# A Silu table load ahead of the output copies, and packed transposes one block later, in an attention and two-layer feed-forward kernel

## The chip, the core and the metric

The kernel runs on one core of one Trainium2 chip. The metric is the device time of one execution in microseconds (us). The core has TensorE (PE in the profile, the matrix engine), VectorE (DVE), ScalarE (ACT), GpSimd (POOL) and SyncE (SP, which here only issues DMAs). Each engine works through its own instructions in order, and waits on semaphores that other engines raise.

## What is computed

```python
def sm_attn(qq, kk, vv):
    s = scale * np.matmul(qq, kk.transpose(0, 1, 3, 2))
    s = s - np.max(s, axis=-1, keepdims=True)
    a = np.exp(s)
    a = a / (np.sum(a, axis=-1, keepdims=True) + 1e-09)
    return np.matmul(a, vv)
p_packed = sm_attn(p, k, v)             # 32 packed rows attend to 576 tokens
out = sm_attn(q, p_packed, p_packed)    # 576 tokens attend to the 32 packed rows
...
rms = np.sqrt(np.mean(x * x, axis=-1, keepdims=True) + 1e-06)
xn = x / rms * rms_g
g = xn @ w_gate
silu = g * (1.0 / (1.0 + np.exp(-g)))
val = xn @ w_val
x = silu * val @ w_out                  # first feed-forward layer, d_ff 1536
...
h = x @ w_in
g = np.maximum(h, 0.0) + alpha * np.minimum(h, 0.0)
return g @ w_out                        # second layer, d_ff 2048
```

There are 8 batches, 8 heads, 576 tokens of 64 dims a head, so 4608 tokens of model width 512. Everything is float32.

## The kernel before, in words

There are two stages. Stage one (about 50 to 810 us of the trace, after a prologue for batch 0) runs attention and the first feed-forward layer. Stage two runs the second layer, and the change does not touch it.

Stage one is a sequence of 16 token tiles, two halves (half 0 and half 1, 288 tokens each) for each of the 8 batches. A tile runs over 12 blocks f = 0 to 11 of 128 hidden units. Each wide product is made of three matmul passes (high and low parts, lines 476 to 478). For a block PE does

- the gate product: 6 matmuls, an_hi/an_lo against m_hi/m_lo, into one PSUM bank;
- the value product: 6 more into another bank;
- the down product of block f - 2: 12 matmuls, h_hi/h_lo against ow_hi/ow_lo, into four banks.

After the 12 blocks two more down products (of blocks 10 and 11) finish a tile. ACT makes Silu of the gate (line 851) once the gate product is done; DVE multiplies it with the value product (line 1050, called the multiply below); ACT rounds the result to h_hi (line 857); DVE makes the rest h_lo (line 1053). There is one gate bank and one value bank, so PE may start the gate product of block f only when Silu of f - 1 is done (`silu_done`), and the value product of f only when the multiply of f - 1 is done (`h32_done`). At the end of a tile DVE copies two output banks (line 1061) and ACT two (lines 865 and 867).

Beside tile (batch b, half) the attention of batch b + 1 is made in small pieces. The order is written out by hand in three tables, PE_PLACES, DVE_PLACES and ACT_PLACES. A key such as (0, "between", 4) means: in half 0, at block 4, at the hook "between". On PE "after" lies between the value product of a block and the down product, and "between" behind the down product. On DVE and ACT "within" lies ahead of the block's first instruction, "after" behind the multiply or Silu, and "between" behind h_lo or h_hi. The last batch has nothing beside it. The pieces that matter here:

- `exp0`, `exp1` on ACT: Exp over the packed scores, behind Silu of block 3 in half 0. `norm0`, `norm1` on DVE divide by the sums (line 932 last).
- `turn_a01` on PE: 8 transposes of those probabilities (line 510), which wait for `norm1` (`a_normed`). They fill banks 2 and 3. `turn_a0` on ACT (line 773) and `turn_a1` on DVE (line 938) copy them out. `turn_a2` on PE, behind the down product of block 5, is 2 more transposes into bank 2, and waits for the copy of `turn_a0` (`at_act`).
- `probs` on ACT in half 0 at block 11: Exp of the second attention. `sums0`, `probs0`, `turn_p0` on DVE at the start of half 1 finish it.
- `fold0` to `fold5` and `x0` to `x3` in half 1: PE products for the next batch's m and x. `x0` (line 575) waits for `m_lo_done`, which DVE raises at line 1010. ACT makes m_hi at line 818.
- `rsqrt0`, `rsqrt1` on ACT in half 1: Ln and Exp.

Exp and Ln use another ACT function table than Silu. A table is loaded by an ACT_TABLE_LOAD instruction; where the program has none, one is put in front of the first activation that needs the other table (the loads at lines 851, 764 and 783). At each of the first 14 tile ends Exp was the last function used, so a load for Silu stands in front of the next tile's first Silu.

Of the kernel before, what the change touches and what calls it, by code (L numbers as in the profile page):

```python
# [40 lines left out]
PE_PLACES = {  # L41
    (0, "ready", 1): ["scores0_ready"], (0, "after", 1): ["scores0"],
    (0, "ready", 2): ["scores1_ready"], (0, "after", 2): ["scores1"],
    (0, "between", 4): ["turn_a01"], (0, "between", 5): ["turn_a2"], (0, "between", 6): ["packed"],
    (0, "after", 7): ["turn_packed"],
# [8 lines left out]
}  # L54
DVE_PLACES = {
    (0, "between", 2): ["max0", "max1"], (0, "between", 3): ["norm0"],
    (0, "within", 4): ["norm1"], (0, "within", 5): ["turn_a1"], (0, "within", 7): ["packed"],
# [8 lines left out]
}  # L66
ACT_PLACES = {
    (0, "between", 1): ["scores0"], (0, "between", 2): ["scores1"], (0, "after", 3): ["exp0", "exp1"],
    (0, "after", 5): ["turn_a0"], (0, "within", 6): ["turn_a2"],
    (0, "within", 8): ["packed"], (0, "after", 11): ["probs"],  # L70
# [3 lines left out]
}  # L74
FILLERS = {"scores0": 3, "scores1": 1, "turn_a01": 2, "packed": 1, "turn_packed": 1, "tokens0": 1, "tile": 6}

# [1 line left out]
def build(nc, q_t, k_t, v_s, p_t, w1_gv, w1_o, w2, rms_g, alpha, out_t):  # L78
# [3 lines left out]
    with ExitStack() as ctx:  # L82
# [127 lines left out]
        def first(c):  # L210

            return isinstance(c, int) and c == 0
# [540 lines left out]
        def _(act):  # L753
            def scores_copy(c, h):

                act.wait_ge(scores_mm, 2 * c + h + 1)
                if h == 0:
                    reached(act, a2n_done, 2 * c)
                nc.scalar.copy(a_sb[:, :, h * HALF:(h + 1) * HALF], scores_ps).then_inc(scores_out, 1)

            def scores_exp(c, g):

                act.wait_ge(bias1_done, GROUPS * c + g + 1)
                nc.scalar.activation(a_sb[:, g, :], a_sb[:, g, :], ACT.Exp, bias=bias1[:, g:g + 1],
                                     scale=SCALE, accum_out=sum1[:, g:g + 1]).then_inc(exp1_done, 1)

            def turn_a(c, t):
                if t == 0:
                    reached(act, mean_mm, 2 * c)
                act.wait_ge(at_mm, 3 * c + t + 1)  # L770
                rows = slice(0, P) if t == 0 else slice(LAST, P)
                dst = a_t[rows, 2 * t:min(2 * t + 2, CHUNKS), :]
                nc.scalar.copy(dst.rearrange("p j n -> p (j n)"), at_ps[t][rows, :]).then_inc(at_act, 1)

            def packed(c):
                act.wait_ge(ppt_mm, c + 1)
                reached(act, s2_mm, 2 * c)
                reached(act, ppg_done, c)
                nc.scalar.copy(flat(pp_t[:]), ppt_ps).then_inc(ppt_copied, 1)

            def probs(c):
                act.wait_ge(sub2_done, 2 * c + 2)
                nc.scalar.activation(flat(e2[:].rearrange("p h g s -> p h (g s)")), flat(e2[:].rearrange("p h g s -> p h (g s)")),
                                     ACT.Exp, scale=SCALE).then_inc(exp2_done, 2)

            def probs_half(c, h):
                act.wait_ge(sub2_done, 2 * c + h + 1)
                nc.scalar.activation(e2[:, h], e2[:, h], ACT.Exp, scale=SCALE).then_inc(exp2_done, 1)

            def tokens_out(c, i):  # L790
                act.wait_ge(x_mm, 4 * c + i + 1)
                if i == 2:
                    act.wait_ge(mean_mm, 2 * c + 1)
                at = x_bank(c, i)
                nc.scalar.activation(sq[:, 2 * (i % 2):2 * (i % 2) + 2, :], psum[:, at:at + 2, 0:HALF],
                                     ACT.Square).then_inc(squared, 1)

            def rsqrt(c, h):

                nc.scalar.preload_act_table_set("natural_log_exp_and_others")  # L800
                act.wait_ge(mean_copied, 2 * c + h + 1)
                reached(act, a2n_done, 2 * c + h - 1)
                nc.scalar.activation(rinv[:, h, :], mean_sb[:, h, :], ACT.Ln).then_inc(log_done, 1)
                act.wait_ge(log_done, 2 * c + h + 1)
                nc.scalar.activation(rinv[:, h, :], rinv[:, h, :], ACT.Exp, scale=-0.5).then_inc(rsqrt_done, 1)

            def split(c, h):
                act.wait_ge(a2n_done, 2 * c + h + 1)
                if not first(c) and h == 0:
                    act.wait_ge(hidden_mm, NF1 * (2 * c - 1))  # L810
                nc.scalar.copy(an_hi[:, h], a2[:, h]).then_inc(an_hi_done, 1)

            def folded(c, j):
                act.wait_ge(m_mm, NF1 // 2 * c + j + 1)
                if not first(c):
                    act.wait_ge(hidden_mm, NF1 * (2 * c - 1) + 2 * j + 2)
                for e in range(2):
                    nc.scalar.copy(m_hi[:, 2 * j:2 * j + 2, e, :],
                                   psum[:, m_bank(c, j) + e, :].rearrange("p (f n) -> p f n", f=2)).then_inc(m_hi_done, 1)

            def beside(c, name):
                if name in ("scores0", "scores1"):
                    scores_copy(c, int(name[-1]))
                if name in ("exp0", "exp1"):
                    scores_exp(c, int(name[-1]))
                if name in ("turn_a0", "turn_a2"):
                    turn_a(c, int(name[-1]))
                if name == "packed":
                    packed(c)
                if name == "probs":  # L830
                    probs(c)
                if name in ("probs0", "probs1"):
                    probs_half(c, int(name[-1]))
                if name[0] == "x":
                    tokens_out(c, int(name[1:]))
                if name[:4] == "fold":
                    folded(c, int(name[4]))
                if name in ("rsqrt0", "rsqrt1"):
                    rsqrt(c, int(name[-1]))
                if name == "split0":  # L840
                    split(c, 0)

            def tile(b, half, at):
                n = 2 * b + half
                for f in range(NF1):
                    at("within", f)
                    act.wait_ge(gate_mm, NF1 * n + f + 1)
                    if f >= SLOTS:

                        act.wait_ge(h_lo_done, NF1 * n + f - 2)  # L850
                    nc.scalar.activation(act_sb[:, f % SLOTS, :], gate_ps, ACT.Silu).then_inc(silu_done, 1)  # L851
                    at("after", f)
                    act.wait_ge(h32_done, NF1 * n + f + 1)
                    if f >= SLOTS:

                        act.wait_ge(down_mm, NF1 * n + f - 2)
                    nc.scalar.copy(h_hi[:, f % SLOTS, :], act_sb[:, f % SLOTS, :]).then_inc(h_hi_done, 1)  # L857
                    at("between", f)
                    if half == 0 and f == 1:
                        split(b, 1)  # L860


                act.wait_ge(y_stored, 16 * n + 16)
                act.wait_ge(out_mm, (KC - 1) * n + 3)
                nc.scalar.copy(y_sb[:, 2, :], y_ps(2)).then_inc(y_act, 1)
                act.wait_ge(down_mm, NF1 * n + NF1)
                nc.scalar.copy(y_sb[:, 3, :], y_ps(3)).then_inc(y_act, 1)  # L867
                at("end", 0)

            nc.scalar.preload_act_table_set("natural_log_exp_and_others")  # L870
            for name in ("scores0", "scores1", "exp0", "exp1", "turn_a0", "turn_a2", "packed", "probs0", "fold0", "probs1",
                         "fold1", "fold2", "x0", "x1", "fold3", "rsqrt0", "x2", "x3", "split0", "fold4", "fold5", "rsqrt1"):
                beside(0, name)
            tiles_of_a(act, tile, beside)


# [247 lines left out]
```

## Time and profile before

| | |
|---|---|
| median of 3 runs | 1603.03 us (1602.67 to 1603.18) |
| profiled execution | 1600.78 us, of it the span of the trace 1599.0 us |
| PE busy | 1563.8 us, 98% of the span |
| DVE busy | 730.1 us, 46% |
| ACT busy | 489.3 us, 31% |
| POOL busy | 206.8 us, 13% |
| chain of work that ended last | PE 91%, DVE 4%, ACT 4%, issue 1% |
| PE clock granted | 0.995 on the mean; 8 tenths in the first of 40 slices, 9 or more after |

The engines are asynchronous, so a busy share says who works most, and not yet where time is lost. The lost time is in the idle stretches of PE, and the view that groups waits names who ended each. Start times are counted from the span's start. A matmul's listed length overlaps the next one's; in steady work one of 288 columns starts every 0.13 us.

### The profile page before, as it was taken

How to read it: one execution, taken by the hardware profiler on the slowest of the kernel's cores; microseconds unless marked ns; L12 is line 12 of the kernel's file. 1: busy time of each engine (PE TensorE's matmuls, PEld its weight loads, DVE VectorE, ACT ScalarE, POOL GpSimd, SP SyncE). 2: the span in 40 equal slices, each digit the busy share in tenths (PEclk: the TensorE clock that was granted, in tenths of full speed). 3: DMA queues.
4: the chain of work that ended last, by engine and by line, in shares of the span. 5: the costliest groups of instructions: out<-in, count | busy, mean ns of one | idle time of the engine just before them, and what ended most of it. 6: DMA issues, size and time to landing. Idle time of an engine off the chain costs nothing.

```text
span 1599.0 us, 25845 instructions
## 1 busy us (share of the span) xinstructions
PE 1563.8 (98%) x10390; PEld 1317.3 (82%) x10390; DVE 730.1 (46%) x1264; ACT 489.3 (31%) x913; POOL 206.8 (13%) x148
## 2 busy tenths in 40 slices
PE   6999999999999999999999999999999999999998
PEld 2788888888888888979988888888888888888887
DVE  5554454554545454454453434443443434343343
ACT  3445454463545535454211111111111111111111
POOL 1701010010100001012680101010100101010000
PEclk8999999999999999999999999999999999999999
DMA  9112102121030211103130101000000001010000
GB/s 358 63 45 76 46 1 77 45 77 45 2 106 16 77 46 32 45 16 147 42 121 0 53 0 52 0 26 26 26 26 15 38 0 52 0 52 0 20 7 27
DMA packets 38627, 76.18 MB, mean 48 GB/s; under 512 B 2192, under 2 KB 11408, under 8 KB 38544
## 3 DMA queue, kind: packets, MB, share of 16 engines
q1 hardware_dynamic: 33360, 65.55, 12.0%
q10 hardware_dynamic: 5184, 9.44, 1.5%
q8 instruction: 62, 1.02, 0.3%
q14 instruction: 21, 0.17, 0.0%
HBM read 56.11 MB, written 18.87 MB: 47 GB/s over the span
## 4 chain that ended last, share of the span: by engine, by line
PE 91%; DVE 4%; ACT 4%; issue 1%; POOL 0%; ACTq 0%; DVEq 0%; POOLq 0%
PE psum L476 29%; PE psum L477 27%; PE psum L478 27%; PE psum L606 2%; PE psum L575 1%; ACT L851 1%; PE psum L691 1%; PE psum L497 1%; DVE h_lo L1053 1%; PE psum L510 1%; DVE m_lo L1010 1%; PE psum L523 1%; PE psum L548 1%; ACT h_hi L857 1%; DVE a_sb L932 1%
## 5 line engine op out<-in xcount | busy, mean ns | idle before, releaser
L1086 DVE TENSOR_TENSOR h_lo<-g,h_hi 128x512 fp32r<-128x512 f32 x144 | 126.1, 876 | 451.4 <-ACT h_hi L884 451.4
L884 ACT CAST h_hi<-g 128x512 fp32r<-128x512 f32 x144 | 89.4, 621 | 638.5 <-PE psum L478 570.6
L476 PE MATMUL psum<-an_hi,m_hi 128*128 128x288 f32 x768 | 236.6, 308 | 10.7 <-ACT act_sb L851 9.4
L476 PE MATMUL psum<-h_hi,ow_hi 128*128 128x288 f32 x768 | 235.4, 306 | 0.0
L477 PE MATMUL psum<-h_hi,ow_lo 128*128 128x288 f32 x768 | 227.2, 296 | 0.0
L477 PE MATMUL psum<-an_hi,m_lo 128*128 128x288 f32 x768 | 226.7, 295 | 0.0
L478 PE MATMUL psum<-h_lo,ow_hi 128*128 128x288 f32 x768 | 225.9, 294 | 0.0
L478 PE MATMUL psum<-an_lo,m_hi 128*128 128x288 f32 x768 | 225.8, 294 | 0.0
L476 PEld LDWEIGHTS psum<-an_hi,m_hi 128*128 128x128 f32 x768 | 144.0, 187 | 43.3 <-issue 33.7
L1050 DVE TENSOR_TENSOR act_sb<-act_sb,psum 128x288 f32<-128x288 f32 x192 | 87.0, 453 | 199.4 <-PE psum L478 160.0
L476 PEld LDWEIGHTS psum<-h_hi,ow_hi 128*128 128x128 f32 x768 | 144.1, 188 | 34.8 <-issue 33.5
L1053 DVE TENSOR_TENSOR h_lo<-act_sb,h_hi 128x288 fp32r<-128x288 f32 x192 | 105.2, 548 | 101.1 <-ACT h_hi L857 100.5
L477 PEld LDWEIGHTS psum<-h_hi,ow_lo 128*128 128x128 f32 x768 | 144.6, 188 | 0.4
L477 PEld LDWEIGHTS psum<-an_hi,m_lo 128*128 128x128 f32 x768 | 144.4, 188 | 0.6 <-issue 0.2
L478 PEld LDWEIGHTS psum<-h_lo,ow_hi 128*128 128x128 f32 x768 | 144.5, 188 | 0.0
L478 PEld LDWEIGHTS psum<-an_lo,m_hi 128*128 128x128 f32 x768 | 144.4, 188 | 0.0
L476 PE MATMUL psum<-xs,w_hi_front 128*128 (+1 forms) x360 | 140.1, 389 | 0.5 <-ACT y_sb L867 0.5
L476 PE MATMUL psum<-h_hi,w_hi_front 128*128 128x512 f32 x360 | 140.6, 391 | 0.0
L477 PE MATMUL psum<-h_hi,w_lo_front 128*128 128x512 f32 x360 | 140.1, 389 | 0.0
L478 PE MATMUL psum<-h_lo,w_hi_front 128*128 128x512 f32 x360 | 140.1, 389 | 0.0
L477 PE MATMUL psum<-xs,w_lo_front 128*128 (+1 forms) x360 | 140.0, 389 | 0.0
L478 PE MATMUL psum<-xs,w_hi_front 128*128 (+1 forms) x360 | 140.0, 389 | 0.0
(123 smaller groups left out, 2422.5 us busy)
## 6 DMA issues: line engine op xcount, KB each, us to landing
k_sb<-k_t SPq DMA_DIRECT2D x16, 576.0 KB, 4.8
q_sb<-q_t SPq DMA_DIRECT2D x8, 1152.0 KB, 5.9
y_mid<-y_sb SPq DMA_DIRECT2D x16, 576.0 KB, 3.4
xs_raw<-y_mid SPq DMA_DIRECT2D x9, 1024.0 KB, 5.4
out_t<-o_sb ACTq DMA_DIRECT2D x36, 256.0 KB, 2.0
v_sb<-v_s SPq DMA_DIRECT2D x8, 1024.0 KB, 6.5
gv_sb<-w_gv SPq DMA_DIRECT2D x4, 1536.0 KB, 18.3
w_raw_front<-w SPq DMA_DIRECT2D x2, 2560.0 KB, 13.0
```

The source lines that it names most:

```text
L476: nc.tensor.matmul(dst, w_hi, hi, start=start, stop=False)
L477: nc.tensor.matmul(dst, w_lo, hi, start=False, stop=False)
L478: return nc.tensor.matmul(dst, w_hi, lo, start=False, stop=stop)
L497: mm = nc.tensor.matmul(scores_ps[PACK * pair:PACK * (pair + 1), e, :], p_sb[dims, pair, :], k_sb[dims, pair, h * HALF:(h + 1) * HALF], st ...
L510: mm = nc.tensor.transpose(at_ps[t][:, at:at + P], a_sb[:, g, KEY_STARTS[j]:KEY_STARTS[j] + P], ident[:])
L523: mm = nc.tensor.matmul(pp_ps[PACK * pair:PACK * (pair + 1), e * HEAD_DIM:(e + 1) * HEAD_DIM], a_t[:, j, col:col + PACK], v_sb[:, j, head ...
L548: mm = nc.tensor.matmul(s2_ps(e)[PACK * pair:PACK * (pair + 1), :], pp_t[dims, pair, :], q[dims, pair, h * HALF:(h + 1) * HALF], start=Tru ...
L606: mm = nc.tensor.matmul(psum[keys, m_bank(c, j) + e, :].rearrange("p (f n) -> p f n", f=2), pp_tg[dims, pair, :], gv_sb[dims, 2 * j:2 * j ...
L884: nc.scalar.copy(h2_hi[:, f % 2, :], g32[:, f % 2, :]).then_inc(g_hi_done, 1)
L1050: nc.vector.tensor_tensor(act_sb[:, s, :], act_sb[:, s, :], val_ps, ALU.mult).then_inc(h32_done, 1)
L1053: nc.vector.tensor_tensor(h_lo[:, s, :], act_sb[:, s, :], h_hi[:, s, :].bitcast(F32), ALU.subtract).then_inc(h_lo_done, 1)
L1086: nc.vector.tensor_tensor(h2_lo[:, s, :], g32[:, s, :], h2_hi[:, s, :].bitcast(F32), ALU.subtract).then_inc(g_lo_done, 1)
```

## The change

There are three edits.

1. PE: `turn_a01` moves from behind the down product at block 4 to between the value and the down product at block 5. The two copies that empty it follow: on DVE from ahead of the multiply of block 5 to behind h_lo of block 5, on ACT from between Silu and h_hi of block 5 to behind h_hi.
2. ACT: a new piece `silu` at the end of block 11 in both halves issues the load of the Silu table.
3. `beside` on ACT gets the branch for it.

```diff
 PE_PLACES = {
-    (0, "between", 4): ["turn_a01"], (0, "between", 5): ["turn_a2"], (0, "between", 6): ["packed"],
+    (0, "after", 5): ["turn_a01"], (0, "between", 5): ["turn_a2"], (0, "between", 6): ["packed"],
...
 DVE_PLACES = {
-    (0, "within", 4): ["norm1"], (0, "within", 5): ["turn_a1"], (0, "within", 7): ["packed"],
+    (0, "within", 4): ["norm1"], (0, "between", 5): ["turn_a1"], (0, "within", 7): ["packed"],
...
 ACT_PLACES = {
-    (0, "after", 5): ["turn_a0"], (0, "within", 6): ["turn_a2"],
-    (0, "within", 8): ["packed"], (0, "after", 11): ["probs"],
+    (0, "between", 5): ["turn_a0"], (0, "within", 6): ["turn_a2"],
+    (0, "within", 8): ["packed"], (0, "after", 11): ["probs"], (0, "between", 11): ["silu"],
...
-    (1, "between", 9): ["x3"], (1, "within", 10): ["fold4", "split0"], (1, "between", 11): ["rsqrt1", "fold5"],
+    (1, "between", 9): ["x3"], (1, "within", 10): ["fold4", "split0"], (1, "between", 11): ["rsqrt1", "fold5", "silu"],
...
+                if name == "silu":
+                    nc.scalar.preload_act_table_set("silu_and_others")
```

ACT at the end of a half 0 and the start of half 1, in the program before (y_sb is the output copy, act_sb is Silu):

```order
L783 ACT_TABLE_LOAD [waits sub2_done]
L783 ACTIVATE e_59<-e_59 128x1152
L857 CAST h_hi<-act_sb 128x288 [waits down_mm,h32_done]
L865 COPY y_sb<-psum 128x288 [waits out_mm,y_stored]
L867 COPY y_sb<-psum 128x288 [waits down_mm]
L851 ACT_TABLE_LOAD
L851 ACTIVATE act_sb<-psum 128x288 [waits gate_mm]
```

The same place in the changed program:

```order
L783 ACT_TABLE_LOAD [waits sub2_done]
L783 ACTIVATE e_59<-e_59 128x1152
L859 CAST h_hi<-act_sb 128x288 [waits down_mm,h32_done]
L843 ACT_TABLE_LOAD
L867 COPY y_sb<-psum 128x288 [waits out_mm,y_stored]
L869 COPY y_sb<-psum 128x288 [waits down_mm]
L853 ACTIVATE act_sb<-psum 128x288 [waits gate_mm]
```

The load has moved ahead of the two copies; the number of rows is the same (two lines were added above, so numbers from 842 on are 2 higher). At the end of half 1 it stands in the same way behind the two m_hi casts of `fold5`.

PE around `turn_a01` in the program before (h_lo against ow_hi ends a down product, an_hi against m_hi begins a gate product):

```order
L478 MATMUL psum<-h_lo,ow_hi 128x288
L510 MATMUL psum<-ident,a_sb 128x128 [waits a_normed]
L510 MATMUL psum<-ident,a_sb 128x128 x7
L476 MATMUL psum<-an_hi,m_hi 128x288 [waits silu_done,m_lo_done]
L477 MATMUL psum<-an_hi,m_lo 128x288
```

The same in the changed program:

```order
L478 MATMUL psum<-an_lo,m_hi 128x288
L510 MATMUL psum<-ident,a_sb 128x128 [waits a_normed]
L510 MATMUL psum<-ident,a_sb 128x128 x7
L476 MATMUL psum<-h_hi,ow_hi 128x288 [waits h_lo_done,ow_ready]
L477 MATMUL psum<-h_hi,ow_lo 128x288
```

The 12 matmuls of the gate and value product of block 5 now stand ahead of the 8 transposes.

## Rows read from the trace of the kernel before

**Rows 1.** Waits of PE: engine, line, waited for, us in total, times, longest.
```profile
PE psum L476 <- ACT act_sb L851: 9.4, 14, 0.7
...
PE psum L510 <- DVE a_sb L932: 5.3, 8, 2.6
...
PE psum L575 <- DVE m_lo L1010: 1.8, 7, 0.3
```

**Rows 2.** Timeline, ACT, end of half 0: start, length, instruction, idle before.
```profile
190.44 0.42 ACT L857 CAST h_hi<-act_sb 128x288 fp32r<-128x288 f32 x1
193.02 0.40 ACT L865 COPY y_sb<-psum 128x288 f32<-128x288 f32 x1 [2.16 <-PE psum L478]
...
193.78 1.28 ACT L851 ACT_TABLE_LOAD   x1
195.07 0.41 ACT L851 ACTIVATE act_sb<-psum 128x288 f32<-128x288 f32 x1
```

**Rows 3.** Timeline, PE, blocks 0 and 1 of the following half 1.
```profile
194.62 0.29 PE L478 MATMUL psum<-an_lo,m_hi 128*128 128x288 f32 x1
195.53 0.40 PE L476 MATMUL psum<-an_hi,m_hi 128*128 128x288 f32 x1 [0.62 <-ACT act_sb L851]
195.77 0.30 PE L477 MATMUL psum<-an_hi,m_lo 128*128 128x288 f32 x1
```

**Rows 4.** Timeline, ACT, end of half 1.
```profile
241.33 1.07 ACT L818 CAST m_hi<-psum 128x512 fp32r<-128x512 f32 x2
244.30 0.40 ACT L865 COPY y_sb<-psum 128x288 f32<-128x288 f32 x1 [1.89 <-PE psum L478]
...
245.06 1.28 ACT L851 ACT_TABLE_LOAD   x1
```

**Rows 5.** Timeline, PE, blocks 0 and 1 of the following half 0.
```profile
245.89 0.29 PE L478 MATMUL psum<-an_lo,m_hi 128*128 128x288 f32 x1
246.91 0.37 PE L476 MATMUL psum<-an_hi,m_hi 128*128 128x288 f32 x1 [0.72 <-ACT act_sb L851]
```

**Rows 6.** Timeline, PE, blocks 0 and 1 of the last tile, which has no load.
```profile
771.10 0.29 PE L478 MATMUL psum<-an_lo,m_hi 128*128 128x288 f32 x1
771.24 0.30 PE L476 MATMUL psum<-an_hi,m_hi 128*128 128x288 f32 x1
...
772.03 0.38 PE L476 MATMUL psum<-an_hi,m_hi 128*128 128x288 f32 x1
772.26 0.30 PE L477 MATMUL psum<-an_hi,m_lo 128*128 128x288 f32 x1
```

**Rows 7.** Timeline, DVE, the multiply of block 0 in that last tile.
```profile
771.51 0.46 DVE L1050 TENSOR_TENSOR act_sb<-act_sb,psum 128x288 f32<-128x288 f32 x1 [1.95 <-PE psum L478]
```

**Rows 8.** Timeline, DVE: batch 1's block 4, and the start of a half 1.
```profile
65.87 0.44 DVE L1050 TENSOR_TENSOR act_sb<-act_sb,psum 128x288 f32<-128x288 f32 x1
...
195.51 0.46 DVE L1050 TENSOR_TENSOR act_sb<-act_sb,psum 128x288 f32<-128x288 f32 x1 [2.45 <-ACT act_sb L851]
...
200.83 1.25 DVE L1010 TENSOR_TENSOR m_lo<-psum,m_hi 128x512 fp32r<-128x512 f32 x2
```

**Rows 9.** Timeline, PE, x0 in that half 1.
```profile
202.23 0.71 PE L575 MATMUL psum<-a,pp 32*64 32x288 f32 x8 [0.26 <-DVE m_lo L1010]
```

**Rows 10.** Timeline, PE, turn_a01 for batch 1 and for a later batch.
```profile
66.00 1.09 PE L510 MATMUL psum<-ident,a_sb 128*128 128x128 f32 x8 [0.94 <-DVE a_sb L932]
...
162.55 0.29 PE L478 MATMUL psum<-h_lo,ow_hi 128*128 128x288 f32 x1
163.13 1.09 PE L510 MATMUL psum<-ident,a_sb 128*128 128x128 f32 x8 [0.29 <-DVE a_sb L932]
163.98 0.38 PE L476 MATMUL psum<-an_hi,m_hi 128*128 128x288 f32 x1
```

**Rows 11.** Timeline, ACT, Silu of block 4 and the copy of turn_a0.
```profile
162.26 0.41 ACT L851 ACTIVATE act_sb<-psum 128x288 f32<-128x288 f32 x1
...
165.36 0.58 ACT L773 COPY a_t<-psum 128x512 f32<-128x512 f32 x1
```

## The prediction

> **What bounds the kernel now.** I read the page first: PE is busy for 98% of the span and makes up 91% of the chain that ended last, while DVE and ACT are under half busy. So time can only be won where PE stands still. The second view was the list of PE's waits. The reader is to see in it [rows 1] that PE waits for Silu at 14 places, 9.4 us in all, that the transposes of line 510 wait 8 times for DVE's normalized probabilities (one is the prologue's with 2.6 us, which the change leaves alone; 7 lie in the tiles), and that x0 waits 7 times for m_lo, 1.8 us. The third view was the timeline around each of these. The 14 waits for Silu are the tile boundaries of batches 0 to 6: 7 from half 0 to half 1 (0.62 each) and 7 from half 1 to half 0 (0.72), all alike to 0.01 us. ACT makes two output copies, loads the table in 1.28 us and only then makes Silu of block 0 [rows 2], which PE needs for its gate product of block 1 [rows 3, 5].
>
> **Edit 2, the load, at the boundary from half 1 to half 0.** Before, the last value matmul of block 0 starts at 245.89 and the next gate product at 246.91 [rows 5]. Steady work would have taken 0.13, so 1.02 - 0.13 = 0.89 us are lost. After the edit the load stands behind the m_hi casts, which end at 241.33 + 1.07 = 242.40, and ends at 243.68. ACT's next work, the output copy, starts only at 244.30 because it waits for PE [rows 4]. So the load is hidden by ACT's own idle time, with 0.6 us to spare. What is late next? The last tile shows it, since it has no load: gate product of block 1 at 771.24, which is 0.14 behind the last value matmul at 771.10, so no wait, and the value product of block 1 at 772.03, 0.79 later and again without one to speak of; its second matmul starts 0.23 instead of 0.13 later [rows 6]. A PE that resumes after Silu shows the same stretch (195.53 to 195.77) [rows 3], so it stands on both sides of the sum and I leave it out. Later waits don't take the 0.89 back until block 4, since all pieces there are started by PE and move with it. 7 x 0.89 = 6.2 us. The bounds are the idle time that the profile names (7 x 0.72 = 5.0) and the loss with the stretch added (7 x 0.99 = 6.9).
>
> **Edit 2 at the boundary from half 0 to half 1.** PE loses 195.53 - 194.62 - 0.13 = 0.78 us here [rows 3]. The load moves behind the h_hi cast, which ends at 190.86, so it ends at 192.14, and the copy starts at 193.02 [rows 2]: hidden, with 0.88 to spare. But PE doesn't keep the whole 0.78. At the start of half 1 DVE has a full list: multiply and h_lo of block 0, sums0, probs0, multiply and h_lo of block 1, turn_p0, m_lo. From the multiply at 195.51 to the end of m_lo at 202.08 [rows 8] it pauses twice only, 0.5 us each, and each time for an h_hi cast that itself answers DVE's multiply. PE's x0 already waits 0.26 us for the end of this list [rows 9]. So this list sets the time of x0, and it moves only as far as its first multiply does. Before, that one waited for Silu (2.45 us idle, ended by ACT) [rows 8]. After, it waits for the value product. In the last tile it starts 771.51 - 771.10 = 0.41 us behind the last value matmul [rows 6, 7], which gives 194.62 + 0.41 = 195.03 here, 0.48 earlier. So PE wins 0.48 and the wait at x0 grows by 0.30. 7 x 0.48 = 3.4 us. Bounds: 7 x 0.3 = 2.1, if the list loses another 0.2, and 7 x 0.78 = 5.5, if it doesn't bind.
>
> **A rule on the load's price.** In these rows every load takes 1.28 us and the next activation starts 0.01 behind it [rows 2]. The Trainium skill, "ScalarE: Activation LUTs", section "What ACT_TABLE_LOAD costs", says that a switch is 1283 ns of load and about 1380 ns of drain, 2.66 us in all. By that figure the load would outlast the idle time at both boundaries; by the rows it doesn't. The trace agrees with the load's length and shows no drain behind it. I go by the rows and keep the other as a part of a rival below.
>
> **Edit 1, turn_a01.** Before, the last matmul of the down product starts at 162.55 and the transposes at 163.13, so 0.58 - 0.13 = 0.45 us are lost to `a_normed` [rows 10]; this is so 6 times (idle 0.29 or 0.30). After, the gate product of block 5 stands there. It needs Silu of block 4, which ends at 162.26 + 0.41 = 162.67 [rows 11], and PE arrives at 162.68. At the boundaries Silu's end reaches PE 0.05 later (195.07 + 0.41 = 195.48 to 195.53) [rows 2, 3] or 0.15 later (245.06 + 1.29 + 0.41 = 246.76 to 246.91) [rows 4, 5]. So a new wait of 0.04 to 0.14 comes in, say 0.1, and a stretch of 0.1 behind it. The transposes themselves come 1.6 us later, when norm1 (ahead of 163.1) is long done; their own length is the same. Left: 0.45 - 0.2 = 0.25, times 6 is 1.5 us. Batch 1 has a longer wait (0.94 idle) [rows 10], where GpSimd works beside DVE. There the next thing late is the value product of block 5, which needs the multiply that ends at 65.87 + 0.44 = 66.31 [rows 8]. PE would reach that product about 65.9, so it waits 0.45 of the 1.1 us that it lost; with two stretches 0.4 us are won. Edit 1 gives 1.9 us; bounds 0 and 7 x 0.45 = 3.2.
>
> **What queues behind the moved pieces.** On ACT the copy of turn_a0 now stands behind h_hi of block 5, and PE's turn_a2 waits for it. Counted from the start of the last value matmul of block 5: the multiply starts at 0.41 [rows 6, 7] and takes 0.46, h_hi 0.42, the copy 0.58 [rows 2, 8, 11], with handovers about 1.95. PE gets to turn_a2 at 0.13 + 0.85 for the transposes (163.13 to 163.98) [rows 10] + 12 x 0.13 + a stretch of 0.1 = 2.65. So 0.7 us are left, and I price this at nothing. DVE's turn_a1 is behind h_lo of block 5 and is needed a block later, at `packed`. The number of table loads doesn't change (60 in all), no DMA is moved, and SP's and POOL's queues are untouched.
>
> **The sum.** 6.2 + 3.4 + 1.9 = 11.5 us. The profiled execution took 1600.78 us (span 1599.0 and 1.8 around it), so it would take 1589.3. The median of the timed runs is 2.25 us above the profiled one, which I take to stay: 1603.03 - 11.5 = 1591.5 us.
>
> **The rivals.**
>
> *The DVE list does not bind.* Then PE wins 0.78 at each of the 7 boundaries into half 1, 2.1 us more: 1589.4. For it speaks that the wait at x0 is only 0.26 us; against it, that the list has no pause that PE or a late ACT piece fills. Chance 0.12.
>
> *Edit 1 wins nothing,* because the wait for `a_normed` turns into one for Silu of block 4 of the same length. The two ends lie 0.4 us apart and the arrival of PE is within 0.01 of Silu's end, so a little more delay in the Exp chain ahead of it eats the gain. 1591.5 + 1.9 = 1593.4. Chance 0.12.
>
> *The load outlasts the gap.* If a load that comes straight behind a cast cost twice its row, 2.57 us, it would end at 244.97 at the end of half 1, the two copies at 245.7, Silu at 246.14, and PE would go on at about 246.24 instead of 246.02: 0.22 lost 7 times. In half 0 it ends at 193.43, the copies at 194.2, and Silu starts by then anyway. 1591.5 + 1.5 = 1593.0. The skill's page above would speak for this; the rows, with 0.01 us between load and Silu, against. Chance 0.05.
>
> *Slower: turn_a2 waits for the copy.* The place is the down product of block 5 in half 0. It decides from a copy that is 0.7 us later than worked out. To make the kernel slower by more than 0.2% it must cost (11.5 + 3.2) / 7 = 2.1 us a batch, so the copy would have to come 2.8 us late, which gives some 1606. Nothing on ACT's list there is that long, since both table loads of this half are done by block 4. Chance 0.02.
>
> **How the numbers follow.** My forecast has 0.67, the rivals 0.12, 0.12, 0.05 and 0.02, and 0.02 is left for no change, where each gap closed opens another. All but the last two are faster. A measurement of this kernel can tell a difference from about 0.2%, that is 3.2 us, so I give 0.96 for faster, 0.02 for the same and 0.02 for slower. The range: all lower bounds together are 5.0 + 2.1 + 0 = 7.1 us won (1595.9), all upper bounds 6.9 + 5.5 + 3.2 = 15.6 (1587.4). They won't all come together; I take 1588.0 to 1595.8.
>
> **What the profile after would show.** Right: 14 table loads at the new line between the last cast of block 11 and the first output copy, Silu of block 0 directly when the gate product is done, and PE's waits for Silu down from 9.4 us in 14 places to under 1 us, most of it now at block 5 of half 0. The first multiply of half 1 is ended by PE and not by ACT, and PE's wait for m_lo at x0 rises from 1.8 to about 4 us. The wait of line 510 for DVE is left in the prologue alone. Wrong: output copies that start behind a load instead of behind PE; a wait of PE at turn_a2 for line 773; a wait at x0 that stays at 0.26 us, which would mean that the list did not bind; or a step that holds back PE in block 1 to 3 of half 0, so that the 0.89 is not kept.

## The result, and the profile after

The changed kernel takes 1590.03 us (median of 4 runs, 1588.93 to 1593.56) against 1602.85 us (4 runs) for the kernel before. The ratio is 0.9927, 95% interval 0.9908 to 0.9946, so 8.7 to 14.7 us were won; the prediction was 11.5, and 1591.5 us for the median.

The profiled execution is the slowest of the four, 1593.56 us with a span of 1591.8, only 7.2 us shorter than the one before, where 1589.3 us was predicted for it. The missing 4 us arise before any instruction that the change touches. The first gate product of the first tile starts at 49.99 us before and at 53.96 after, and the prologue ahead of it is the same code. The view by stretches shows where; its columns are the stretch, its length, busy us and count of PE, PEld, DVE, ACT, POOL, then the granted clock of PE, the DMA share and GB/s. The kernel before:

```profile
45.00:50.00 5.00, 5.00 (x15) 2.32 (x13) 3.08 (x7) 3.09 (x4) 0.72 (x1) 1.00 0.00 0
50.00:55.00 5.00, 5.00 (x46) 4.10 (x45) 1.50 (x4) 1.75 (x5) 4.84 (x6) 1.00 0.02 3
```

The changed kernel:

```profile
45.00:50.00 5.00, 4.43 (x6) 2.19 (x7) 3.88 (x8) 3.98 (x6) 0.51 (x1) 0.50 0.01 3
50.00:55.00 5.00, 5.00 (x14) 2.46 (x13) 0.12 (x1) 0.00 (x0) 4.64 (x5) 0.83 0.00 0
```

The granted clock is at its lower level, 1.2 GHz, from 45 to 50 us, and 0.83 on the mean from 50 to 55, where the kernel before had the full 2.4 GHz: 3.0 of the 4.0 us. The other 0.9 is there at the first matmuls on k (6.98 and 7.90 us). So all that follows is measured from the first gate product of the tiles to the first matmul of the second layer: 760.28 us before and 749.03 after, 11.25 us won. The second layer takes 788.7 us before and 788.8 after.

PE's waits in the changed kernel (engine, line, waited for, us, times, longest; line numbers past 842 are 2 higher than before):

```profile
PE psum L476 <- DVE act_sb L1052: 3.7, 9, 1.2
PE psum L510 <- DVE a_sb L934: 2.6, 1, 2.6
...
PE psum L575 <- DVE m_lo L1012: 1.8, 7, 0.3
```

Against [rows 1] the 14 waits for Silu (9.4 us) are gone, and line 510 waits in the prologue alone. In their place stand 9 waits for the multiply on DVE, 3.7 us: 7 of 0.22 to 0.23 us at the start of half 1, one of 0.91 in batch 1 and one of 1.22 in the last tile. The kernel before had only the last of these, 1.3 us. The wait of x0 is as it was.

The end of half 0 on ACT, which answers to [rows 2] (start, length, instruction, idle before):

```profile
192.96 0.42 ACT L859 CAST h_hi<-act_sb 128x288 fp32r<-128x288 f32 x1
193.39 1.28 ACT L843 ACT_TABLE_LOAD   x1
195.53 0.40 ACT L867 COPY y_sb<-psum 128x288 f32<-128x288 f32 x1 [0.85 <-PE psum L478]
195.87 0.40 ACT L869 COPY y_sb<-psum 128x288 f32<-128x288 f32 x1
196.66 0.41 ACT L853 ACTIVATE act_sb<-psum 128x288 f32<-128x288 f32 x1 [0.40 <-PE psum L478]
```

The end of half 1 on ACT, which answers to [rows 4]:

```profile
244.44 1.28 ACT L843 ACT_TABLE_LOAD   x1
246.31 0.40 ACT L867 COPY y_sb<-psum 128x288 f32<-128x288 f32 x1 [0.59 <-PE psum L478]
...
247.45 0.41 ACT L853 ACTIVATE act_sb<-psum 128x288 f32<-128x288 f32 x1 [0.39 <-PE psum L478]
```

Both loads lie in ACT's idle time with 0.85 and 0.59 us to spare (0.88 and 0.6 were predicted), and Silu of block 0 waits for PE and no longer for a table. PE at the start of that half 1, which answers to [rows 3, 9]:

```profile
197.13 0.29 PE L478 MATMUL psum<-an_lo,m_hi 128*128 128x288 f32 x1
197.26 0.30 PE L476 MATMUL psum<-an_hi,m_hi 128*128 128x288 f32 x1
...
200.82 0.29 PE L478 MATMUL psum<-an_lo,m_hi 128*128 128x288 f32 x1
201.33 0.40 PE L476 MATMUL psum<-an_hi,m_hi 128*128 128x288 f32 x1 [0.22 <-DVE act_sb L1052]
...
204.24 0.71 PE L575 MATMUL psum<-a,pp 32*64 32x288 f32 x8 [0.26 <-DVE m_lo L1012]
```

No wait is left ahead of block 1: its gate product starts 0.13 us behind the last value matmul of block 0 (197.13 to 197.26). A wait of 0.22 us is listed at the value product of block 2 (201.33), which the multiply of block 1 releases, and x0 waits its old 0.26. DVE in the same place, which answers to [rows 8]:

```profile
197.53 0.45 DVE L1052 TENSOR_TENSOR act_sb<-act_sb,psum 128x288 f32<-128x288 f32 x1 [1.96 <-PE psum L478]
...
200.83 0.45 DVE L1052 TENSOR_TENSOR act_sb<-act_sb,psum 128x288 f32<-128x288 f32 x1
...
202.85 1.25 DVE L1012 TENSOR_TENSOR m_lo<-psum,m_hi 128x512 fp32r<-128x512 f32 x2
```

The first multiply is now released by PE. From there to the start of m_lo it is 5.32 us, as it was before (195.51 to 200.83).

The wait at the value product of block 2 is new in the list, but the dependence was there. The same place in the kernel before, PE and the multiply of block 1 on DVE:

```profile
198.81 0.45 DVE L1050 TENSOR_TENSOR act_sb<-act_sb,psum 128x288 f32<-128x288 f32 x1
```
```profile
199.11 0.29 PE L478 MATMUL psum<-an_lo,m_hi 128*128 128x288 f32 x1
199.31 0.40 PE L476 MATMUL psum<-an_hi,m_hi 128*128 128x288 f32 x1
```

The value product started 0.05 us behind the end of the multiply (199.26) and 0.20 behind the last gate matmul, so 0.07 late, which the view of waits does not name. In the changed kernel it again starts 0.05 behind the multiply's end (201.28), and 0.51 behind the gate matmul. PE is 0.31 us later here than before.

PE around the moved transposes, which answers to [rows 10]:

```profile
165.37 0.29 PE L478 MATMUL psum<-h_lo,ow_hi 128*128 128x288 f32 x1
165.64 0.37 PE L476 MATMUL psum<-an_hi,m_hi 128*128 128x288 f32 x1
165.84 0.30 PE L477 MATMUL psum<-an_hi,m_lo 128*128 128x288 f32 x1
...
167.30 1.04 PE L510 MATMUL psum<-ident,a_sb 128*128 128x128 f32 x8
```

The gate product of block 5 comes 0.27 after the down product instead of 0.13, so 0.14 late, and its next matmul 0.07 late. The transposes wait for nothing.

Where the time went, from the start times of the same piece in both traces (after minus before; only the change from row to row counts):

| piece | before | after | shift | won since the row above |
|---|---|---|---|---|
| scores0, half 0 | 151.51 | 154.33 | +2.82 | |
| packed | 170.78 | 173.29 | +2.51 | 0.31 (edit 1) |
| fold0, half 1 | 197.32 | 199.04 | +1.72 | 0.79 (load) |
| x0 | 202.23 | 204.24 | +2.01 | -0.29 (given back) |
| scores0 of the next half 0 | 248.66 | 249.81 | +1.15 | 0.86 (load) |

The later batches win 1.67 to 1.69 us each. The first stretch, from scores0 of batch 1 to scores0 of batch 2, wins 1.14, read below under batch 1.

### The profile page after: what moved, and what is told of

The parts are those of the page before. It is cut to its first block, busy times and chain, and to the rows that moved or that the text cites. A ratio compares the mean times of both kernels' runs of the same rounds, so it can differ in the third digit from the quotient of the medians.

```text
span 1591.8 us, 25845 instructions
## 1 busy us (share of the span) xinstructions
PE 1566.0 (98%) x10390; PEld 1319.4 (83%) x10390; DVE 727.9 (46%) x1264; ACT 487.7 (31%) x913; POOL 206.2 (13%) x148
## 4 chain that ended last, share of the span: by engine, by line
PE 94%; DVE 3%; ACT 1%; issue 1%; POOL 0%; ACTq 0%; DVEq 0%; POOLq 0%
PE psum L476 30%; PE psum L477 28%; PE psum L478 28%; PE psum L606 2%; PE psum L575 1%; PE psum L691 1%; PE psum L497 1%; DVE m_lo L1012 1%; PE psum L523 1%; PE psum L548 1%; PE psum L584 1%; PE psum L510 1%; DVE h_lo L1055 1%; DVE act_sb L1052 0%; ACT h_hi L859 0%
```

## The experiments

All eight ran beside the kernel before. "Tiles" is the stretch from the first gate product to the second layer in the profiled execution.

| run | edit | median us | ratio to before (95%) | tiles us |
|---|---|---|---|---|
| before | | 1602.9, 1602.4 | | 760.28 |
| changed | | 1590.03 | 0.9927 (0.9908 to 0.9946) | 749.03 |
| e1_load_only | load alone | 1593.37 | 0.9936 (0.9916 to 0.9955) | 751.24 |
| e2_turns_only | transposes alone | 1600.57 | 0.9983 (0.9972 to 0.9995) | 757.86 |
| e3_two_loads | changed, loads doubled | 1591.81 | 0.9926 (0.9910 to 0.9943) | 749.23 |
| e4_sums_early | changed, sums0 earlier | 1585.07 | 0.9890 (0.9874 to 0.9907) | 742.62 |
| f4_after_again | changed, again | 1591.96 | 0.9931 (0.9914 to 0.9947) | 748.98 |
| f5_pool_pause | changed, GpSimd paused | 1590.01 | 0.9920 (0.9904 to 0.9937) | 747.98 |
| f3_sums_on_before | before, sums0 earlier | 1598.04 | 0.9972 (0.9962 to 0.9983) | 756.70 |
| f1_best | all together | 1583.02 | 0.9877 (0.9861 to 0.9894) | 740.48 |

**One edit at a time.** e1_load_only:

```diff
-    (0, "within", 8): ["packed"], (0, "after", 11): ["probs"],
+    (0, "within", 8): ["packed"], (0, "after", 11): ["probs"], (0, "between", 11): ["silu"],
...
-    ... (1, "between", 11): ["rsqrt1", "fold5"],
+    ... (1, "between", 11): ["rsqrt1", "fold5", "silu"],
```

> The kernel before with the Silu load at the end of block 11 and nothing else. Theory (the two edits add up): each boundary into half 1 wins 0.50 us, each into half 0 wins 0.86, 14 boundaries, so 9.5 us, and line 510 still waits 0.3 us for a_normed 6 times. Time about 1593.3 if before is 1602.8. Rival (the load is worth nothing without the later transposes, because the wait for a_normed takes the time back): the wait at line 510 grows to about 1.1 us a batch and the kernel wins 3.5 us only.

The tiles are 9.04 us shorter. A batch takes 95.75 us (154.23 to 249.98) against 97.15 before, so 1.40 each, where 1.36 was expected; batch 1 gave some of it back (below). Line 510 waits 5.9 us in 8 places, the prologue's 2.6 among them. The median, 1593.37 us, is within 0.1 us of the forecast. The rival is out.

e2_turns_only:

```diff
-    (0, "between", 4): ["turn_a01"],     # PE
+    (0, "after", 5): ["turn_a01"],
-    (0, "within", 5): ["turn_a1"],       # DVE
+    (0, "between", 5): ["turn_a1"],
-    (0, "after", 5): ["turn_a0"],        # ACT
+    (0, "between", 5): ["turn_a0"],
```

> The kernel before with the transposes and their two copies one block later and nothing else. Theory: 0.30 us won a batch in 6 batches, batch 1 between -0.3 and +0.4 depending on how GpSimd's work falls on VectorE's, so 1.5 to 2.2 us; the 14 waits for Silu stay at 9.4 us. Rival (the transposes only win once the load is gone): under 0.3 us in all.

The tiles are 2.42 us shorter, a little above the range: 0.34 a batch and 0.39 in batch 1. The 14 waits for Silu are still 9.4 us. So edit 1 wins without edit 2. 9.04 + 2.42 = 11.46 against 11.25 for both: they add up to 0.2 us.

**The price of a load.** e3_two_loads:

```diff
                 if name == "silu":
+                    nc.scalar.preload_act_table_set("natural_log_exp_and_others")
                     nc.scalar.preload_act_table_set("silu_and_others")
```

> The changed kernel with a second, useless table load (for Ln and Exp) ahead of each of the 14 loads, so 2.57 us of loads in the gap that has 2.13 us at the end of half 0 and 1.87 at the end of half 1. Theory (a load costs its 1.28 us and nothing else): the output copies of ACT start 0.4 to 0.7 us late, Silu of block 0 is 0.05 us late in half 1 and 0.3 us late in half 0, PE waits 0.2 to 0.3 us at 7 places, and the kernel is 1.5 to 2.1 us slower than the changed one. Rival (each load also drains, 2.66 us as the Trainium skill says in ScalarE: Activation LUTs, What ACT_TABLE_LOAD costs): the second load adds 2.66, Silu is about 3 us late at every boundary and the kernel is over 25 us slower.

The two loads at the end of a half 1, on ACT:

```profile
241.28 1.08 ACT L818 CAST m_hi<-psum 128x512 fp32r<-128x512 f32 x2
242.37 1.28 ACT L843 ACT_TABLE_LOAD   x1
243.66 1.28 ACT L844 ACT_TABLE_LOAD   x1
244.96 0.40 ACT L868 COPY y_sb<-psum 128x288 f32<-128x288 f32 x1
245.25 0.41 ACT L870 COPY y_sb<-psum 128x288 f32<-128x288 f32 x1
245.54 0.43 ACT L854 ACTIVATE act_sb<-psum 128x288 f32<-128x288 f32 x1
```

A cast, two loads and a copy follow each other with 0.01 us between them, and each load takes its 1.28. A load that costs double is out here; so is the drain of about 1380 ns that the Trainium skill gives in "ScalarE: Activation LUTs", section "What ACT_TABLE_LOAD costs", while its 1283 ns for the load itself is what every load here shows. My own figure for the delay was too high too. PE waits a little:

```profile
245.84 0.29 PE L478 MATMUL psum<-an_lo,m_hi 128*128 128x288 f32 x1
246.12 0.37 PE L476 MATMUL psum<-an_hi,m_hi 128*128 128x288 f32 x1
```

That is 0.28 instead of 0.13, and a batch takes 95.57 us (152.30 to 247.87) against 95.48: 0.1 us, not 0.2 to 0.3. The copies, when late, follow each other 0.29 us apart, where I had taken 0.4. The tiles are 0.20 us longer, since batch 1 happened to run 0.6 us better here, and the median, 1591.81, lies between the two of the changed kernel, where 1.5 to 2.1 us more were expected. So the changed order has room for a second load almost free.

**DVE's list at the start of half 1.** e4_sums_early:

```diff
-    (0, "after", 10): ["shift1"],
-    (1, "between", 0): ["sums0"], (1, "within", 1): ["probs0"], ...
+    (0, "after", 10): ["shift1"], (0, "between", 11): ["sums0"],
+    (1, "within", 1): ["probs0"], ...
```

> The changed kernel with sums0 on VectorE (1.2 us: a reduction and two small operations) moved from behind block 0 of half 1 to behind block 11 of half 0, where VectorE is idle. Theory (VectorE's list at the start of half 1 holds PE back): the 0.22 us wait of the value product of block 2 and the 0.26 us wait of x0 both go, 0.5 to 0.7 us a batch, 3.5 to 4.9 us faster than the changed kernel. Rival (the list does not bind, PE itself does): no more than 0.5 us in all.

The tiles are 6.41 us shorter than in the changed kernel: 0.81 a batch by x0's place, more than expected, and 0.6 in batch 1 from the way GpSimd's work falls there (below). The expectation added the listed waits, 0.22 and 0.26, and these understate the loss. By start times the value product of block 2 stood 0.51 us behind the last gate matmul and now stands 0.13 behind it, its second matmul is no longer 0.10 late, and x0 stood 0.56 behind the down product and now 0.22: 0.38 + 0.10 + 0.34 = 0.82. In PE's waits the line for x0 is gone and the one for the multiply has two places left:

```profile
PE psum L476 <- DVE act_sb L1052: 1.6, 2, 1.3
```

f3_sums_on_before has the same edit on the kernel before.

> The kernel before with only sums0 moved to the end of half 0. Theory (before the change PE lost 0.78 us to Silu at the boundary into half 1, and VectorE's list cost it only what came on top): 0.81 us a batch is what this move gives the changed kernel, and 0.30 of it is what the list took from the load's gain, so here it gives 0.5 us a batch, 3.3 to 3.9 us in all. Rival (the list was as costly before): 0.8 a batch, 5.6 us.

By x0's place, as above, it wins 0.51 us a batch (a whole batch takes 96.61 us, 153.17 to 249.78, against 97.15), and the tiles are 3.58 us shorter. So the same move is worth 0.30 us a batch more once Silu comes early. This difference, and the 0.29 us that x0 gives back in the table, are two measurements of one thing: what DVE's list took from the load's gain.

**Batch 1.** In the changed kernel's trace the value product of block 5 in the first tile waits 0.91 us. PE, DVE and POOL there:

```profile
70.94 0.40 PE L476 MATMUL psum<-an_hi,m_hi 128*128 128x288 f32 x1 [0.91 <-DVE act_sb L1052]
```
```profile
67.17 1.07 DVE L1055 TENSOR_TENSOR h_lo<-act_sb,h_hi 128x288 fp32r<-128x288 f32 x1 [1.95 <-ACT h_hi L859]
...
69.36 1.16 DVE L934 TENSOR_SCALAR a_sb<-a_sb,rcp 128x576 f32<-128x576 f32 x1
70.45 0.44 DVE L1052 TENSOR_TENSOR act_sb<-act_sb,psum 128x288 f32<-128x288 f32 x1
```
```profile
66.65 1.28 POOL L438 TENSOR_TENSOR ow_lo<-ow_raw,ow_hi 128x512 fp32r<-128x512 f32 x1
...
68.80 1.41 POOL L438 TENSOR_TENSOR ow_lo<-ow_raw,ow_hi 128x512 fp32r<-128x512 f32 x1
```

h_lo takes 1.07 instead of 0.46 and the last norm 1.16 instead of 0.52, each while GpSimd's subtraction runs. f5_pool_pause takes that away:

```diff
             for f in range(NF1):
+                if f == 5:
+                    pool.wait_ge(hidden_mm, 6)
```

> The changed kernel, with GpSimd held at its sixth split of the output weights until PE has done the value product of block 5 of the first tile, so that no split runs beside batch 1's Exp, norms and multiply. Theory (batch 1 wins less because VectorE's operations stretch beside GpSimd's): the 0.91 us wait of the value product of block 5 in batch 1 goes, and the first tile is 0.5 to 1.0 us shorter; the other batches don't change. Rival (the wait is Silu's or the table load's): no change.

The two operations in f5_pool_pause, on DVE (the start of the tiles is 0.8 us earlier):

```profile
66.37 0.46 DVE L1057 TENSOR_TENSOR h_lo<-act_sb,h_hi 128x288 fp32r<-128x288 f32 x1 [2.11 <-ACT h_hi L861]
...
67.95 0.52 DVE L936 TENSOR_SCALAR a_sb<-a_sb,rcp 128x576 f32<-128x576 f32 x1
68.38 0.45 DVE L1054 TENSOR_TENSOR act_sb<-act_sb,psum 128x288 f32<-128x288 f32 x1
```

Both are back at 0.46 and 0.52, PE has no wait there, and the tiles are 1.05 us shorter, just above the range; the other batches take what they took. The ends of the stretched operations tell more. In the changed kernel's trace 15 of the h_lo subtractions in the tiles take over 0.6 us, and every one of them ends 0.31 or 0.32 us behind the end of a GpSimd cast or subtraction; the stretched norm (end 70.52, GpSimd's 70.21) does too. So how long such an operation takes is set by how much of GpSimd's instruction is still ahead when it starts.

How much batch 1 loses thus depends on how the two engines' work falls together, and the low clock of the prologue shifts it. GpSimd's first subtraction of the output weights starts 1.3 us behind the first gate product in six traces (51.32 against 49.99 in the kernel before) and 1.7 us ahead of it in the four that start latest (52.23 against 53.96 in the changed kernel): there PE came 4.0 us later and GpSimd 0.9. From scores0 to packed of batch 1 the traces give

| GpSimd's first subtraction | without edit 1 | with edit 1 |
|---|---|---|
| behind (tiles start at 49.8 to 52.4 us) | 19.91 (before), 19.94 (f3) | 19.52 (e2), 19.53 (e3), 19.52 (e4) |
| ahead (tiles start at 53.5 to 54.0 us) | 20.51 (e1) | 20.13 (changed), 20.13 (again) |

In a like alignment edit 1 wins 0.39 or 0.38 us, and the late one costs 0.6. With the pause the same stretch takes 18.97 us in f5_pool_pause (ahead) and 18.95 in f1_best (behind), as in every later batch, so GpSimd costs batch 1 1.16 us in one alignment and 0.57 in the other.

**The changed kernel again.** f4_after_again:

> The changed kernel once more, as the base of its neighbours here. Theory: everything from the first tile on repeats to 0.1 us (749.0 us from the first gate product to the second stage, 0.6 less where batch 1 falls better on GpSimd's work), and whole times differ by the prologue alone, 1588.5 to 1593.5 us. Rival (the first profile's late start comes from the change): the first gate product starts at 54 us again.

The tiles repeat to 0.05 us (748.98), and the waits too. The first gate product started at 53.48, late again, which is what the rival expected. Against the rival stands e4_sums_early, which has the same prologue and both edits and started at 49.95, and e3_two_loads at 52.41. The timed runs of the kernel before spread as widely, from 1600.38 us at a mean granted clock of 0.995 to 1604.66 at 0.992, as those of the changed kernel do (1588.93 at 0.995, 1593.56 at 0.992). So late starts without the change are likely, though no trace of the kernel before shows one. What sets the start of a run (49.8 to 54.0 over the ten profiles) beyond the granted clock in the prologue is open. It is the main spread of the whole times.

**All together.** f1_best is e4_sums_early with the pause of f5_pool_pause and one more:

```diff
             for f in range(W2_FRONT):
+                if f == 6:
+                    pool.wait_ge(hidden_mm, NF1 * (2 * BATCH - 1) + 3)
                 split_w2(f, w2_in[f // (W2_FRONT // 2)])
```

> The changed kernel with sums0 at the end of half 0, the GpSimd pause in the first tile, and a second pause that keeps GpSimd's split of the second layer's weights off blocks 0 to 2 of the last tile (there h_lo took 2.2 us and PE waited 1.2). Theory: 6.4 us from the sums, 0.4 to 1.0 from the first pause and 1.2 to 1.3 from the second, so 8 us faster than the changed kernel, about 1582.5. Rival (GpSimd's later splits then hold up the second stage): a new wait of PE at its first blocks, and no more than 6 us won.

1583.02 us, 1.2% under the kernel before and some 7 to 9 us under the changed one; the tiles are 8.55 us shorter than there. The h_lo of block 0 in the last tile, in the changed kernel:

```profile
765.23 2.20 DVE L1055 TENSOR_TENSOR h_lo<-act_sb,h_hi 128x288 fp32r<-128x288 f32 x1 [0.50 <-ACT h_hi L859]
```

and in f1_best, with GpSimd quiet:

```profile
755.71 0.46 DVE L1059 TENSOR_TENSOR h_lo<-act_sb,h_hi 128x288 fp32r<-128x288 f32 x1 [0.50 <-ACT h_hi L863]
```

PE has no wait for the multiply left, and no new one at the second layer (0.5 us for ACT's copy there, as in the changed kernel), though GpSimd's last split ahead of it starts 21.9 us before the layer, and 27.0 in e4_sums_early.

## Why the prediction was right, point by point

**The load at the boundary into half 0.** 0.89 us predicted, 0.86 to 0.90 measured from x0 to the next scores0 over the batches. The idle time of ACT hid the load. e3_two_loads, where the load outlasts it, shows that there was more room than I had worked out.

**The load at the boundary into half 1.** 0.48 predicted, 0.50 measured (0.79 less 0.29). The cap by DVE's list was the right step: e4_sums_early and f3_sums_on_before differ by 0.30 us a batch for the same edit. But I put the wait in the wrong place. I said that x0's wait would grow from 0.26 to 0.56, and that an unchanged 0.26 would speak against the list. It stayed at 0.26. PE meets the list earlier, at the value product of block 2, which needs the multiply of block 1. There it lost 0.31 us more than before, the size that I had put at x0 (0.30), and from there it runs with the list, so x0 finds it as before. The size came out because both waits hang on the same list. By the prediction's own sign a wait that stays at 0.26 would have meant that the list did not bind; the sign was wrong, the list binds.

**Edit 1.** 0.25 us a batch predicted, 0.31 measured. The new wait for Silu is there with 0.14 (0.04 to 0.14 was said), with a stretch of 0.07 behind it, and is too short for the view of waits to name it. That leaves 0.45 - 0.21 = 0.24. The other 0.06 the sum had put at nothing, with the words that the transposes' own length is the same: behind their wait they took 1.09 us [rows 10], without it 1.04, and the second starts 0.11 behind the first instead of 0.16.

**Batch 1.** 0.4 won predicted, 0.2 lost in the profiled execution. This is the one term with the wrong sign. In a like alignment it is 0.39. The wait for the multiply, which I put at 0.45 us, is listed with 0.30 in e2_turns_only and with 0.91 in the profiled execution, as it depends on where GpSimd's instructions end; I had taken the one trace before as fixed.

**The copy of turn_a0.** Priced at nothing, and no wait appears at turn_a2: in the trace after the copy ends 0.79 us ahead of it, where 0.7 was worked out.

**The sum.** 11.5 predicted for the tiles, 11.25 measured in the profile: 6.2 and 3.4 to 3.5 for the load against 6.2 and 3.4, and 1.65 for edit 1 against 1.9, since batch 1 lost 0.2 instead of winning 0.4 and the six others won 0.06 each more than said. The median of the whole moved by 12.8 us in the first comparison and 10.4 in the later one (1602.39 to 1591.96).

## What to carry to other kernels

Put a table load where its engine waits anyway, ahead of work that needs no special table. When a wait of the busiest engine goes, look for the next engine's list of work that begins at the same event: it moves by less than the wait was long, and shortening it is worth more after the change than before. Where two terms hang on the same list, look for the first instruction that meets it, as the wait shows there and not at the old place. And compare start times besides the list of waits: here waits of 0.07 and 0.14 us were not in it, and the listed 0.22 and 0.26 stood for 0.82 us of PE.

## What the runs showed that I had not expected

Late output copies on ACT run 0.29 us apart, against 0.34 where they are on time (195.53 and 195.87). The same DVE subtraction of 128x288 takes 0.46 us alone, and beside GpSimd it ends 0.31 us behind GpSimd's instruction, which in the tiles of the changed kernel is up to 2.76 us after its own start. And the first 50 us vary by up to 4 us between traces whose prologue is the same code, of which 3 lie, between the two profiles compared here, in how long PE's clock stays at its lower level, so a gain of a few us is better measured from a marker behind the prologue than by the span.
